# Top-32 attention: the two tiles of a pair in turn on VectorE, masks, sines and gatings in a new order

## What is computed

```python
scores = scale * np.matmul(q, k.transpose(0, 1, 3, 2))
kth = np.partition(scores, -top_k, axis=-1)[..., -top_k:-top_k + 1]
scores = np.where(scores >= kth, scores, -1000000000.0)
attn = np.exp(scores - np.max(scores, axis=-1, keepdims=True))
attn = attn / (np.sum(attn, axis=-1, keepdims=True) + 1e-09)
x = np.matmul(attn, v)            # 2304 rows of 512
h = x @ w_in
y = (h * np.cos(h)) @ w_out       # then the experts
...
```

## Time and profile before

| | |
|---|---|
| median of 3 runs | 1412.31 us (1410.16 to 1413.58) |
| profiled execution | 1417.38 us, its span 1415.8 us |
| busy over the span | PE 1266.2 us (89%), DVE 939.5 (66%), ACT 656.0 (46%), POOL 562.1 (40%) |
| last maximum on VectorE | about 918.7 us |
| copy of the scores of loop step 0, 11, 71 | starts at 12.06, 130.56, 895.91 us |
| last copy of attention output (loop step 74) | starts at 942.21 us |

### The profile page before, as it was taken

One profiled execution on the slowest core, in us unless ns is written; L12 is line 12 of the kernel. 1 busy time (PEld: TensorE's weight loads), 2 busy tenths in 40 slices (PEclk: granted clock), 3 DMA queues, 4 the chain that ended last, 5 costly groups with the idle time before them and its releaser, 6 DMA issues. The chain is left out here.

```text
span 1415.8 us, 18220 instructions
## 1 busy us (share of the span) xinstructions
PE 1266.2 (89%) x5962; PEld 803.3 (57%) x5963; DVE 939.5 (66%) x1690; ACT 656.0 (46%) x1082; POOL 562.1 (40%) x696
## 2 busy tenths in 40 slices
PE   4557899989999999899899999899399999999996
PEld 2435656856747747648658558476244444444443
DVE  6999998999999999999999999905211111111110
ACT  3455665666666766665766756624011111111110
POOL 2444463364563564654454554614411111111111
PEclk9567999999999999999999999999699999999999
DMA  8301001101001100100010000003034442243000
GB/s 245 95 8 25 1 8 33 42 8 40 1 9 41 41 8 16 25 8 16 19 47 16 1 16 1 1 16 127 24 136 150 147 150 103 73 167 128 15 13 1
DMA packets 81839, 71.52 MB, mean 51 GB/s; under 512 B 62266, under 2 KB 62266, under 8 KB 81248
## 3 DMA queue, kind: packets, MB, share of 16 engines
q1 hardware_dynamic: 76192, 60.86, 13.4%
q0 software_dynamic: 5568, 9.65, 2.2%
HBM read 62.97 MB, written 11.45 MB: 53 GB/s over the span
## 5 line engine op out<-in xcount | busy, mean ns | idle before, releaser
L720 DVE MAX8 tops<-scores_left 128x8 f32<-128x576 f32 x432 | 327.3, 758 | 12.3
L407 POOL TENSOR_TENSOR probs<-scores,probs 128x576 f32<-128x576 f32 x144 | 211.0, 1465 | 244.1 <-ACT probs L514 244.1
L976 PE MATMUL dense_banks<-x_T,weights 128*128 128x256 f32 x1024 | 246.4, 396 | 16.6 <-ACT h_T L552 16.6
L986 PE MATMUL dense_banks<-weights,h_T 128*128 128x512 f32 x512 | 236.6, 605 | 0.0
L976 PEld LDWEIGHTS dense_banks<-x_T,weights 128*128 128x128 f32 x1024 | 196.6, 197 | 58.0 <-ACT h_T L552 20.0
L723 DVE MATCH_REPLACE8 scores_left<-tops,scores_left 128x576 f32<-128x576 f32 x288 | 213.9, 743 | 0.0
L1128 PE MATMUL dense_banks<-weights,expert_h_T 128*128 x400 | 183.8, 592 | 0.0
L1109 PE MATMUL score_banks<-weights,x_gathered_T 128*128 x400 | 182.1, 598 | 1.0 <-DVE x_gathered_T L864 1.0
L514 ACT ACTIVATE probs<-scores,top_consts 128x576 f32<-128x576 f32 x144 | 111.5, 775 | 120.9 <-POOL top_consts L404 120.7
L986 PEld LDWEIGHTS dense_banks<-weights,h_T 128*128 128x128 f32 x512 | 93.4, 193 | 106.9 <-issue 106.9
L869 DVE COPY expert_h_T<-dense_banks 128x512 f32<-128x512 f32 x25 | 17.3, 692 | 185.5 <-PE dense_banks L1119 185.5
(11 more groups left out here) (160 smaller groups left out, 1581.3 us busy)
## 6 DMA issues: line engine op xcount, KB each, us to landing
weights<-in_moe_w SPq DMA_DIRECT2D x16, 2048.0 KB, 10.8
y_rows<-y_rows_sb SPq DMA_DIRECT2D x18, 256.0 KB, 2.0
k_rows<-in_k SPq DMA_DIRECT2D x32, 128.0 KB, 2.7
q_rows<-in_q SPq DMA_DIRECT2D x16, 256.0 KB, 3.4
v_rows<-in_v SPq DMA_DIRECT2D x32, 128.0 KB, 2.3
weights<-in_moe_w_in SPq DMA_DIRECT2D x1, 4096.0 KB, 13.0
weights<-in_moe_w_out SPq DMA_DIRECT2D x1, 4096.0 KB, 22.4
k_rows<-in_k SPq DMA_DIRECT2D x16, 32.0 KB, 2.6
```

Source lines behind the costliest of these rows:

```text
L407: nc.gpsimd.tensor_tensor(ex, SS[:, u % 3, i, :], ex, ALU.subtract).then_inc(s["masked_done"], 1)
L720: V.max(top, src).then_inc(s["tops_done"], 1)
L976: last = MM(HO[:, f % 2, 0:BT], win[:, kd, f * P:(f + 1) * P], XT[:, m % 2, kd, :], start=kd == 0, stop=kd == KD - 1)
L986: last = MM(HO[:, t, :], HS[:, f, t * P:(t + 1) * P], wout[:, f, :], start=f == 0, stop=f == NF - 1)
```

## The change

VectorE takes the operations of the two tiles in turn: operation 0 of tile 0, operation 0 of tile 1, operation 1 of tile 0 and so on, with a second buffer of leftover scores (`WK` has two tiles). An operation waits for the one of its own tile, two places ahead. The reciprocals stand between the last maxima of tile 0 and tile 1; the two halves of a reduction stand behind operations 1 and 2. VectorE works on pair st in loop step st, and ScalarE and GpSimd do both tiles' masks of pair st-1 in step st. The values stay three pairs behind (`LAG` is 3 in both).

```diff
+def tops_at(u, i, op):
+    return 14 * u + 2 * op + i + 1
...
-        WK = sb("scores_left", [P, S], stack=att)
+        WK = sb("scores_left", [P, 2, S], stack=att)
...
             for st in range(LOOP):
-                u = st - 2
+                u = st - 1
                 if 0 <= u < NS:
+                    mask(u, 0)
                     mask(u, 1)
-                gate(st, 0)
...
+                gate(st, 0)
                 gate(st, 1)
-                if 0 <= st - 1 < NS:
-                    mask(st - 1, 0)
-                gate(st, 2)
...
+                gate(st, 2)
                 gate(st, 3)
...
+                if 0 <= st - 1 < NS:
+                    below(st - 1, 0)
+                    below(st - 1, 1)
...
+                if 0 <= st - 1 < NS:
+                    exps(st - 1, 1)
+                if 0 <= u < NS:
+                    copy_probs(u)
+                for m, i in dense:
+                    if i in (3, 5):
+                        for h in range(2):
+                            sine(m, (i - 3) // 2, h)
...
-                        sine(m, (i - 2) // 2, 0)
+                        absolute(m, (i - 2) // 2)
...
+                else:
+                    dve.wait_ge(s["tops_done"], tops_at(u, i, op - 1))
+                if op % 2 == 0:
                     V.max(top, src).then_inc(s["tops_done"], 1)
...
             for st in range(LOOP):
...
+                for op in range(7):
+                    for i in range(2):
+                        if st < NS:
+                            top_op(st, i, op)
+                        if op == 6 and i == 0 and 0 <= st - 1 < NS:
+                            reciprocals(st - 1)
+                    for m, i in block_at(st):
+                        if i in (2, 4) and op in (1, 2):
+                            reduce_h(m, (i - 2) // 2, op - 1)
```

More of the change, by code:

```diff
@@ L401, in mask @@
                 a = u % 3
[L402 removed]
+                pool.wait_ge(s["tops_done"], tops_at(u, i, 6))
                 at_least(pool, s["exps_done"], 2 * (u - 3) + i + 1)
@@ L613, in _ @@
                 dense = block_at(st)
-                if 0 <= st - 2 < NS:
-                    below(st - 2, 1)
                 if st < NS:
                     copy_scores(st)
-                for m, i in dense:
-                    if i in (3, 5):
-                        sine(m, (i - 3) // 2, 1)
-                if 0 <= st - 2 < NS:
-                    exps(st - 2, 1)
+                if 0 <= st - 1 < NS:
+                    below(st - 1, 0)
+                    below(st - 1, 1)
                 for m, i in dense:
@@ L625, in _ @@
                         copy_h(m, 4 * i)
-                        copy_h(m, 4 * i + 1)
-                if 0 <= st - 1 < NS:
-                    below(st - 1, 0)
-                if 0 <= u < NS:
-                    copy_probs(u)
                 if 0 <= st - 1 < NS:
@@ L708, in _, with top_op @@
             V = nc.vector
-            def top_k(u, i):
-                done = (2 * u + i) * 7
-                src = SS[:, u % 3, i, :]
-                if i == 0:
-                    dve.wait_ge(s["scores_copied"], u + 1)
-                at_least(dve, s["consts_done"], 2 * (u - 3) + i + 1)
-                for rnd in range(TOPK // 8):
-                    if i == 1 and rnd == 2 and u >= 1:
-                        reciprocals(u - 1)
-                    top = TOP[:, u % 3, i, rnd * 8:rnd * 8 + 8]
-                    V.max(top, src).then_inc(s["tops_done"], 1)
-                    dve.wait_ge(s["tops_done"], done + 2 * rnd + 1)
-                    if rnd < TOPK // 8 - 1:
-                        V.match_replace(WK[:], top, src, NEG).then_inc(s["tops_done"], 1)
-                        dve.wait_ge(s["tops_done"], done + 2 * rnd + 2)
-                        src = WK[:]
+            def top_op(u, i, op):
+                rnd = op // 2
+                top = TOP[:, u % 3, i, rnd * 8:rnd * 8 + 8]
+                src = SS[:, u % 3, i, :] if op < 2 else WK[:, i, :]
+                if op == 0:
+                    if i == 0:
+                        dve.wait_ge(s["scores_copied"], u + 1)
+                    at_least(dve, s["consts_done"], 2 * (u - 3) + i + 1)
+                else:
+                    dve.wait_ge(s["tops_done"], tops_at(u, i, op - 1))
+                if op % 2 == 0:
+                    V.max(top, src).then_inc(s["tops_done"], 1)
+                else:
+                    V.match_replace(WK[:, i, :], top, src, NEG).then_inc(s["tops_done"], 1)
             def reciprocals(u):
@@ L730, in reciprocals, with reduce_h @@
                 V.reciprocal(RD[:, u % 2, :], DEN2[:, u % 2, :]).then_inc(s["rden_done"], 1)
[L732 to L734 removed]
+            def reduce_h(m, g, part):
                 hs = HS[:, g * 8:(g + 1) * 8, :].rearrange("p a n -> p (a n)")
                 r1 = R[:, g, :, :].rearrange("p a n -> p (a n)")
[L737 to L751 removed]
+                if part == 0:
+                    dve.wait_ge(s["dense_emptied"], m * MOE_FILLS + 8 * (g + 1))
+                    at_least(dve, s["gated_done"], (2 * (m - 1) + g + 1) * 4)
+                    V.tensor_scalar(r1.bitcast(I32), hs, 1.0 / TWO_PI, None, ALU.mult).then_inc(s["reduced_done"], 1)
+                else:
+                    dve.wait_ge(s["reduced_done"], m * 4 + 2 * g + 1)
+                    V.scalar_tensor_tensor(out=r1, in0=r1.bitcast(I32), scalar=-TWO_PI, in1=hs,
+                                           op0=ALU.mult, op1=ALU.add).then_inc(s["reduced_done"], 1)
+            for st in range(LOOP):
+                for op in range(7):
[7 more added lines that the diff above has]
+                            reduce_h(m, (i - 2) // 2, op - 1)
             chain = [0]
```

21 lines of the change are left out of this document (2 added, 19 removed).

## The result

| | before | after |
|---|---|---|
| median | 1412.94 us (1410.16 to 1413.59, 4 runs) | 1507.62 us (1506.29 to 1508.91, 4 runs) |
| span of the profiled execution | 1415.8 us | 1507.3 us |
| copy of the scores of loop step 11, 71 | 130.56, 895.91 us | 144.19, 981.01 us |
| last copy of attention output | 942.21 us | 1037.08 us |

The changed kernel is slower: ratio 1.0674, 95% interval 1.0654 to 1.0694, 95 us. The forecast was 1466 us, in a range of 1405 to 1535. In the spans: +13.6 us up to step 11 (forecast +11), +71.5 from there to step 71 (+37), +9.8 in the tail (+5.6), -3.4 in the rest.

What follows compares the result with a forecast made beforehand. VectorE (95% busy) was taken to set the pace before, and waits through masks and GpSimd after. +37 us in steps 11 to 71, +11 ahead and +5.6 in the tail made +54: 1466 us, range 1405 to 1535.

Steps and rivals of the forecast that it cites:

- rival B: VectorE gains no overlap behind maxima, a pair stays at 11.55 us: 1512 us (1500 to 1535), chance 0.10.
- VectorE's overlap: Tiles in turn on VectorE save about 0.12 us per instruction, so a pair takes 9.8 us instead of 11.55.
- The circle: Masks, probabilities, values, next scores, next Relu: no step can go below about 10.3 us, 10.6 with hidden products.
- i=2: Third step of a block of eight: VectorE carries a reduction and sets the step, 14.45 us.
- i=0, i=1 and i=7: Steps of a block of eight set by the 10.6 us circle plus gates, rows or queries: 12.2, 11.6 and 11.5 us.
- 10.6 with hidden products: Length of the masks' circle in us when TensorE runs hidden products between its scores and the values.
- Gatings and scaling ahead of the constants: On GpSimd, behind the first sine, four gatings and the scaling hold the next pair's constants until 15.4 us.
- i=3: Step with sines and gatings, the next constants then meeting the reduction on VectorE: 16.6 us.
- i=5: Step with sines and gatings like i=3, but without the reduction: 15.6 us.
- i=4: Step with the second reduction: 11.2 us without contention, 13.6 if constants 1 wait for VectorE; taken as 12.9.
- Rival D: TensorE sets the pace, Relu and constants never come late, a step is 10.6 us plus extras: 1344 us, chance 0.16.
- i=6: Step set by the 10.3 us circle plus 0.45 for the table load before the Exps: 10.75 us.

Runs made afterwards that it cites:

- e10: After with Abs and sines on ScalarE back in the places they had before the change: 1451.37 us, ratio 1.0275.
- e9: After with 10 and 7 unused TensorE products ahead of the values in i=4 and i=6: 1496.5 us, ratio 1.0586.
- e2: After, but VectorE takes tile 0 and then tile 1, the reduction between them: 1526.66 us, ratio 1.0777.
- e11: After with constants ahead of subtractions, Abs and sines at their old places, and reduction halves behind operations 4 and 5: 1477.74 us, ratio 1.0397.
- filler: After with unused TensorE products ahead of the values in i=4 and i=6, a longer and a shorter run: 1505.08 and 1496.5 us.
- e7: Before's ScalarE and GpSimd orders; VectorE alternates tiles half a pair apart, reduction and reciprocals moved: 1396.01 us, ratio 0.983 to before.
- e6: Before's ScalarE and GpSimd orders, VectorE's tiles in turn, reciprocals behind operation 6 of tile 0: 1440.32 us, ratio 1.0134 to before.
- e3: After with both tiles' constants on GpSimd behind the previous step's scaling and ahead of its last two gatings: 1443.26 us, ratio 1.0178.
- e4: After with both constants of a pair ahead of both subtractions on GpSimd: 1455.68 us, ratio 1.0265.

## Why the prediction was right, and what it mis-sized

**What was right, and what was luck.** The direction was right, and so were the waits that make after slow. The size was not: +54 us forecast, +95 measured. 1507.62 us lies above the 1440 to 1500 that I gave my own forecast. It lies in the interval of rival B, 4 us from its 1512, and B's condition does not hold, as the next rows show. The time is inside my range only because the range reached up to B's upper end. That is luck: the missing 40 us have causes that I had priced too low or left out, and not the one that I had put at this place.

**VectorE's overlap: right.** The replacements and maxima of after, which wait for nothing in the pipe:

```profile
612.95 0.74 DVE L727 MATCH_REPLACE8 scores_left<-tops,scores_left 128x576 f32<-128x576 f32 x1
613.61 0.08 DVE L727 MATCH_VALUE_LOAD scores_left<-tops,scores_left 128x8 f32 x1
613.68 0.74 DVE L727 MATCH_REPLACE8 scores_left<-tops,scores_left 128x576 f32<-128x576 f32 x1
614.34 1.41 DVE L725 MAX8 tops<-scores_left 128x8 f32<-128x576 f32 x2
```

A replacement or a maximum starts up to 0.08 us before the end of the one ahead, and two maxima take 1.41 together. A pair from 608.78 to 618.50, where the next maximum could start, is 9.7 us long; I had 9.8. Rival B falls. The Trainium skill, "VectorE: DVE Perf Modes", section "The DRAIN you can't avoid", says that nothing is gained by taking semaphores away, and adds that a next operation that is not held starts earlier; the rows bear out the addition and not the first, by 1.8 us a pair.

**The circle: right in i=2, and in i=0 and i=1 right by number.** i=2 is 14.37 us (14.45). i=0, i=1 and i=7 are 12.20, 11.73 and 11.55 us; I had 12.2, 11.6 and 11.5. But TensorE is busy all of that time, so its own work sets these steps and not the masks. My 10.6 with hidden products had TensorE's work in it; I read it as the masks' circle.

**Gatings and scaling ahead of the constants (i=3, i=5): right.** 15.75 and 15.76 us, forecast 16.6 and 15.6. The 1 us of contention that I had added to i=3 did not come there: constants 0 took 0.19 (650.26) and it was constants 1, in i=4, that met the reduction. Rival D, with TensorE setting the pace, falls as a whole: i=3 and i=5 are far above 11 us. In i=0, i=1 and i=7 its condition, a TensorE without gaps, does hold. e10 shows that the sines' place is a large part of what made GpSimd late.

**i=4 and i=6: the failed terms.** Forecast 12.9 and 10.75, measured 15.73 and 12.6. The rows of i=4 in after, from the first Relu at 650.49:

```profile
651.34 1.80 POOL L412 TENSOR_TENSOR probs<-scores,probs 128x576 f32<-128x576 f32 x1 [0.89 <-ACT probs L518]
...
653.09 2.35 POOL L409 TENSOR_TENSOR top_consts<-tops,top_factors 128x2 f32<-128x2 f32 x1
653.12 2.27 DVE L743 SCALAR_TENSOR_TENSOR reduced_h<-reduced_h,h_T 128x2048 f32<-128x2048 int32 x1
...
655.47 0.77 ACT L518 ACTIVATE probs<-scores,top_consts 128x576 f32<-128x576 f32 x1 [4.21 <-POOL top_consts L409]
656.26 1.28 ACT L526 ACT_TABLE_LOAD   x1
...
659.09 1.09 ACT L540 COPY probs_T<-score_banks 128x1152 f32<-128x1152 f32 x1
...
660.24 0.80 PE L966 MATMUL small_banks<-probs_T,v_left 128*128 128x128 f32 x2 [5.52 <-ACT probs_T L540]
660.97 1.98 PE L969 MATMUL small_banks<-probs_T,v_rows 128*64 128x128 f32 x16
662.87 2.29 PE L930 MATMUL score_banks<-k_T,q_T 64*128 64x288 f32 x8
...
663.15 2.00 ACT L584 ACTIVATE reduced_h<-reduced_h 128x1024 f32<-128x1024 f32 x2
...
665.21 1.12 ACT L532 COPY scores<-score_banks 128x1152 f32<-128x1152 f32 x1
```

Three things add to the 11.2 us that I had for i=4 without contention (values, copy of x, two Abs, copy of the scores). The contention comes in full: constants 1 take 2.35 us instead of 0.19, and Relu 1 is at 4.98 on my clock, not 2.45. That is 2.5 us, of which I had allowed 1.7 (12.9 - 11.2). The table load of 1.28 ahead of the Exps, which I had counted only in i=6, adds 0.6: the values start at 9.75 instead of 6.66. And TensorE had idled 5.52 us, and its clock fell to the lower level: the copy of x, which stands ahead of the Abs, starts 2.75 us behind the values (662.99) instead of 1.46 in i=1, which adds 1.3. 11.2 + 2.5 + 0.6 + 1.3 = 15.6. The scores run slower too and are ready at 665.16, but the Abs hold the copy up to 665.15 as well, so this second loss is hidden here. In e9, with the full clock, the product is ready at 652.19 and the copy starts at 653.13, behind the Abs. In i=6, which has no Abs, the walk up to the values held (7.2 against 7.1), and the lower clock adds 0.7 from values to scores and 1.0 from scores to copy. I had priced TensorE's part at full clock, though my own walk left TensorE idle in these steps.

A block has thus 2.8 + 1.85 us more than forecast in i=4 and i=6 and 0.85 less in i=3. In all it is 109.7 instead of 105.6, and seven such blocks make 29 of the 34 us that are missing from steps 11 to 71. Ahead of step 11 a step was 12.7 us, as my circle at the lower clock has it (12.6), where I had mixed in full clock and taken 12.2: 13.6 us instead of 11. The remaining 5 or so and the 4 in the tail (clock 0.88 there instead of 0.96) I did not take apart.

**Prices of the rivals: B's was too high.** I had put the missing overlap at 46 us; e2 cost 12 to 19. Of the 5 us a block that I had for i=0, 1, 2 and 7, 2.6 came: these steps are 12.25, 12.45, 15.24 and 12.49 us in e2, where I had 12.85 and 16.2. The reduction's other place gave 1 back in i=4, and the steps ahead of step 11 cost 4.9 instead of 9. The sines' place I had at about 30 us in the expectation of e10; it was 56. It takes i=4's table load and i=6's lower clock with it, and I had counted neither.

**The causes, by the runs** (each against after): sines at their old place -56 us, both constants first -52 to -58, reduction later -12 to -21, filler -9 to -12, no turns +12 to +19. They don't add, as e11 shows; so the 95 us can't be split among them.

## What to carry to other kernels

Making the busiest engine faster pays only up to the next circle, so walk that circle first, with every instruction that is queued ahead of each link, and with TensorE's clock after the idle time that the walk leaves. Two chains in turn on one engine end together, and so does the work that waits for them: in this kernel it was better to let them end apart (e7, -1.7%) than together (e6, +1.3%), though these two differ in the place of the reduction and the reciprocals as well. Before comparing small changes from run to run, look at a part of the program that none of them touches. Edits that help one at a time can undo each other when one moves a producer later and the other its consumer earlier (e11).

## What was not expected of the hardware

- Constants of 128 x 2 on GpSimd took 2.35 us instead of 0.19 while VectorE ran its scalar_tensor_tensor (653.09 and 653.12 in after), and two subtractions 5.92 beside both halves of the reduction (610.15 in e3) instead of 2.79 away from it (e4). The Trainium skill, "SBUF — State Buffer", section "Who interferes with whom", says that a VectorE instruction with two inputs in SBUF contends with a GpSimd instruction that reads SBUF. The rows agree, and the size of an instruction didn't protect it.
- After 5.52 us without a product TensorE ran the next three groups at about half speed: 0.80, 1.98 and 2.29 us (0.38, 1.09 and 1.24 at the full clock). After 3.39 us in e10 it was the same (0.79, 1.98, 2.29), and after 1.45 us in e10 and 1.51 in e4 it was not (1.09, 1.24).
